# Slot-major pair features, c loaded from 32 outermost rows

## The reference

```python
x = attention(q, k, v)                      # 4608 tokens x 512
logits = x @ phi                            # 32 slots
d = softmax over tokens; slot_input = d.T @ x
slot_out = relu(slot_input[e] @ w1[e]) @ w2[e]      # 8 experts, 4 slots each
c = softmax over slots                      # 4608 x 32
y = c @ slot_out
a = y @ moe2_w1
b = y @ moe2_w2
out = ((a * b) @ moe2_w3) @ moe2_w_out
```

## Time and profile before

| | us |
|---|---|
| median of 3 runs | 410.05 |
| lowest and highest | 409.47, 415.63 |
| the profiled execution | 411.92 |
| its span, first to last instruction | 410.1 |
| PE busy in the span | 377.5 (92%) |
| POOL, DVE, ACT busy | 168.5, 170.8, 125.5 |

### The profile page before, as it was taken

The page is one execution under the profiler, slowest core; times in us unless marked ns, Lnnn a source line. Parts: engine busy times, 40 slices in busy tenths (PEclk is TensorE's granted clock), DMA queues, the critical chain, the costliest instruction groups (busy, mean ns, idle before and its releaser), DMA issues.

```text
span 410.1 us, 10206 instructions
## 1 busy us (share of the span) xinstructions
PE 377.5 (92%) x4215; PEld 272.5 (66%) x4215; DVE 170.8 (42%) x276; ACT 125.5 (31%) x246; POOL 168.5 (41%) x157
## 2 busy tenths in 40 slices
PE   1898989998999799999999999689899999989896
PEld 1887675876877586554545444467688888778775
DVE  1454465555655362530031002699723325532450
ACT  1022312321331134232233212221633435423342
POOL 1243233223322322554444420499645535754470
PEclk9999999999999999999999999899999999999999
DMA  7997999899899959586699980422214444424432
GB/s 261 371 379 245 394 397 342 284 400 390 314 359 378 378 205 339 216 340 268 247 423 419 419 336 2 86 82 95 91 44 157 177 175 176 174 102 176 177 118 102
DMA packets 38088, 102.93 MB, mean 251 GB/s; under 512 B 3552, under 2 KB 7968, under 8 KB 34208
## 3 DMA queue, kind: packets, MB, share of 16 engines
q1 hardware_dynamic: 38048, 102.34, 66.6%
HBM read 92.00 MB, written 10.32 MB: 249 GB/s over the span
## 4 chain that ended last, share of the span: by engine, by line
PE 76%; DMA 9%; issue 4%; POOL 3%; SPq 3%; DVE 3%; ACT 1%; ACTq 0%; DVEq 0%; POOLq 0%
PE psum L957 15%; PE psum L768 12%; PE psum L661 9%; PE psum L783 8%; PE psum L627 8%; DMA c_sb<-c_rows 7%; PE psum L688 5%; PE psum L925 4%; PE psum L647 4%; PE psum L674 4%; PE psum L723 3%; PE psum L699 2%; DMA pkg_sb<-in_tiles 2%; POOL feat L593 2%; SPq L509 2%
## 5 line engine op out<-in xcount | busy, mean ns | idle before, releaser
L593 POOL TENSOR_TENSOR feat<-c_sb 128x512 f32<-128x512 f32 x45 | 62.3, 1408 | 45.8 <-DMA c_sb<-c_rows 29.2
L957 PE MATMUL psum<-m_hi,feat_hi 128*128 128x512 f32 x144 | 56.5, 393 | 5.0 <-ACT out_sb L1124 3.3
L1142 DVE TENSOR_TENSOR weights_t<-psum,const_sb 128x512 f32<-128x512 f32 x72 | 46.3, 685 | 34.5 <-PE psum L627 26.8
L549 POOL TENSOR_TENSOR pkg_sb<-pkg_sb,const_sb 128x512 f32<-128x512 f32 x27 | 28.4, 1052 | 73.4 <-DMA pkg_sb<-in_tiles 73.4
L957 PE MATMUL psum<-m_hi,feat_lo 128*128 128x512 f32 x144 | 56.1, 389 | 0.0
L957 PE MATMUL psum<-m_lo,feat_hi 128*128 128x512 f32 x144 | 56.1, 389 | 0.0
L404 DVE TENSOR_TENSOR feat_lo<-feat,feat_hi 128x512 fp32r<-128x512 f32 x32 | 28.4, 889 | 60.2 <-ACT feat_hi L1092 58.2
L1092 ACT CAST feat_hi<-feat 128x512 fp32r<-128x512 f32 x45 | 27.7, 624 | 55.3 <-POOL feat L593 55.3
L567 POOL TENSOR_TENSOR w_lo<-fold_raw,w_hi 128x512 fp32r<-128x512 f32 x16 | 20.7, 1295 | 49.2 <-ACT wo_hi L1034 49.2
L627 PE MATMUL psum<-pkg_sb 64*64 64x128 f32 (+1 forms) x864 | 27.9, 267 | 10.3 <-DMA pkg_sb<-in_tiles 9.5
L976 ACT COPY state_sb<-psum 128x256 f32<-128x256 f32 x32 | 11.9, 373 | 80.1 <-PE psum L674 80.1
(11 more groups left out here) (136 smaller groups left out, 591.9 us busy)
## 6 DMA issues: line engine op xcount, KB each, us to landing
pkg_sb<-in_tiles SPq DMA_DIRECT2D x57, 256.0 KB, 7.0
pkg_sb<-in_tiles SPq DMA_DIRECT2D x24, 512.0 KB, 7.2
unit_a<-in_units SPq DMA_DIRECT2D x11, 1024.0 KB, 6.9
unit_x<-in_units SPq DMA_DIRECT2D x9, 1024.0 KB, 5.2
c_sb<-c_rows SPq DMA_DIRECT2D x36, 256.0 KB
out<-out_sb SPq DMA_DIRECT2D x36, 256.0 KB, 6.9
fold_raw<-in_fold SPq DMA_DIRECT2D x12, 512.0 KB, 7.2
unit_a<-in_units SPq DMA_DIRECT2D x12, 512.0 KB, 7.7
```

The lines of the kernel that those rows point to most:

```text
L549: nc.gpsimd.tensor_tensor(v_nat(g, t).rearrange("p (h d) -> p h d", h=HEADS), v_nat(g, t).rearrange("p (h d) -> p h d", h=HEADS), decay.un ...
L593: nc.gpsimd.tensor_tensor(feat[:, k, :], c_sb[:, s, x, :], c_sb[:, s, y, :], ALU.mult).then_inc(feat_ready, 1)
L957: last = mm(psum[:, OUT + b, :], x, y, start=(at == 0 and m == 0), stop=(at == 4 and m == 2))
L1142: tt(weights_t[:, (2 * t + odd) % 4, :].rearrange("p (k b n) -> p k b n", k=2, b=2), psum[:, odd, :].rearrange("p (k b n) -> p k b n", k=2 ...
```

## The change

The order of a feature tile's 128 rows is turned round: from four shifts of 32 slots to 32 slots of four shifts, in the tiles 0 to 3; the squares keep their order. `pair_terms` therefore reads and writes runs of four (its source steps are 0, 1 or 2 elements) where it had runs of 32. `load_c` puts the 32 slots outermost in its four loads. The tile with shift 0 now has four copies of each slot side by side, so the squares need a tile of their own in the old order: a fifth load with the shape [4 copies, 32 slots, 512 tokens]. `c_sb` grows by a tile in each buffer, the wait of POOL counts five loads, and the rows that are halved (the shift of 16 counts each pair twice) are now every fourth.

```diff
-        c_sb = place("c_sb", [P, 2, 4, CHUNK * P], at=top[1])
+        c_sb = place("c_sb", [P, 2, 5, CHUNK * P], at=top[1])
...
+        def shifted4(base, at, step, *outer):
+            return bass.AP(base.tensor, base.offset + at,
+                           [list(base.ap[0])] + [list(n) for n in outer] + [[1, SLOTS], [step, 4]])
...
-                (dst[:, 0:2 * P].rearrange("p (k i s) -> p k i s", k=2, s=SLOTS),
-                 shifted(plain, 0, (0, 2), (0, 4)), shifted(y, 1, (1, 2), (2, 4))),
-                (by_slots(dst[:, 2 * P:3 * P]), shifted(plain, 0, (0, 4)), shifted(y, 13, (1, 4))),
-                (by_slots(dst[:, 3 * P:4 * P]), shifted(x, 1, (2, 4)), shifted(y, 13, (1, 4))),
+                (dst[:, 0:2 * P].rearrange("p (k s i) -> p k s i", k=2, s=SLOTS),
+                 shifted4(plain, 0, 0, (0, 2)), shifted4(y, 1, 2, (1, 2))),
+                (dst[:, 2 * P:3 * P].rearrange("p (s i) -> p s i", s=SLOTS),
+                 shifted4(plain, 0, 0), shifted4(y, 13, 1)),
+                (dst[:, 3 * P:4 * P].rearrange("p (s i) -> p s i", s=SLOTS),
+                 shifted4(x, 1, 2), shifted4(y, 13, 1)),
                 (dst[:, 4 * P:NFEAT], shifted(plain, 0), shifted(y, 0))]
...
-        FEATURES = ((0, 1), (0, 2), (0, 3), (1, 3), (0, 0))
+        FEATURES = ((0, 1), (0, 2), (0, 3), (1, 3), (4, 4))
...
+                base = c_rows[:, bass.ds(n * (CHUNK * P), CHUNK * P)]
                 for a, (at, step) in enumerate(C_SHIFTS):
-                    base = c_rows[:, bass.ds(n * (CHUNK * P), CHUNK * P)]
                     src = bass.AP(base.tensor, base.offset + at * TOKENS,
-                                  [[step * TOKENS, 4], [TOKENS, SLOTS], [1, CHUNK * P]])
+                                  [[TOKENS, SLOTS], [step * TOKENS, 4], [1, CHUNK * P]])
                     sp.dma_start(c_sb[:, s, a, :], src).then_inc(c_loaded[s], 16)
+                src = bass.AP(base.tensor, base.offset, [[0, 4], [TOKENS, SLOTS], [1, CHUNK * P]])
+                sp.dma_start(c_sb[:, s, 4, :], src).then_inc(c_loaded[s], 16)
...
-                pool.wait_ge(c_loaded[s], (n + (2 - s)) * 32)
+                pool.wait_ge(c_loaded[s], (n + (2 - s)) * 40)
...
-    c[:, C_HALF] = np.where(np.arange(P) >= 3 * SLOTS, 0.5, 1.0)
+    c[:, C_HALF] = np.where(np.arange(P) % 4 == 3, 0.5, 1.0)
```

## The result

| | before | after |
|---|---|---|
| median, 20 runs each, us | 411.22 | 407.24 |
| lowest and highest | 408.68, 415.63 | 404.52, 409.46 |
| the profiled execution | 411.92 | 409.46 |
| its span | 410.1 | 407.6 |

The ratio of after to before is 0.9899, with a 95% interval of 0.987 to 0.9927: 4.0 us faster, 1%, which is clear of the noise and under the 2% that the prediction took as its line. The forecast was 405.8, with a range of 404.0 to 409.0 and a gain of 4.2. Of the 1.4 us between 405.8 and 407.24, 1.2 lie in the base: three runs of the kernel before gave 410.05, twenty gave 411.22.

The account below looks back on a forecast made before the run. The prediction took four DMA engines' throughput to bound the late chunks, with PE next. Loads -4.2, issue 0, DVE 0 and POOL 0 gave 410.05 - 4.2 = 405.85, rounded to 405.8 us, range 404.0 to 409.0.

Parts of the forecast that it names:

- The bound: Late chunks: throughput of four DMA engines, 328 KB each, 13.1 to 13.4 us a step; PE next with 11.83.
- The gain: Chunk stage, first to last output copy: 98.84 us down to 8 x 11.83 = 94.64, so 4.2 us.
- The wide loads: Chunk stage, four loads with 32 outermost: 402 GB/s as the output stores, 1.05 MB in 2.6 us.
- The bound of 116 GB/s: The four changed loads' bad side, from stores of c in 512 B pieces: 9.0 us a chunk.
- rival C: Loads spread but go slowly, decided near 160 GB/s; over 2% slower 2 in 100, a time between 2 in 100.
- The fifth load: Chunk stage: 262 KB on four engines at 98 GB/s, 2.7 us, hidden by PE's 11.83 us.
- In time: Chunk 3's loads: all there by about 319, POOL can use them about 322.6; about 3.5 us to spare.
- pair_terms: Build of M, runs of four: 0 on DVE (to +0.1 us a slice), 0 on POOL (to +5.5 us).
- Rival A: Build of M: POOL's runs of four are dear; gain given back 8 in 100, over 2% slower 3 in 100.
- its form with a fixed price for each run of four: POOL in pair_terms: each run a read command, 10.9 us a slice, some 55 us slower; 1 in 100.
- The gap ahead of slice 6: Build of M: PE's idle before 287.31, 1.1 us, set by DVE beside POOL's products; called the only gap left.
- rival D: More gain than the stage's, from an earlier first chunk: 405 at best; over 2% faster 2 in 100.

Follow-up runs that it names:

- loaded-up kernel: The changed kernel with its narrow fifth load issued three times, into tiles nobody reads, and waited for: 416.75 us against 411.69 for before, ratio 1.0135.
- five narrow loads: The kernel before with the fifth load alone, all five loads of a chunk with 4 outermost: 428.78 us against 411.69, ratio 1.0438.
- the lists alone: The kernel before with only the new shifted4 and pair_terms (runs of four), loads unchanged: 411.26 us against 410.55, ratio 1.0009.
- two attempts to shrink it: Changed kernel with PE's earlier first-chunk start and chunk 0's first two feature tiles made earlier: 406.25 us; also with the fifth load in four wide parts: 405.95.
- one constant: The changed kernel with PE's first-chunk wait at a count of 2 low parts instead of 5: 403.83 us against 410.55 for before, ratio 0.9842.

## Why the prediction was right

**The bound.** Held. The late steps were the throughput of four DMA engines: 13.15 us at four narrow loads, 15.84 at five, PE's 11.79 at three. The sum of bytes per engine gave 13.1 to 13.4, 15.7 to 16.0, and under 11.79.

**The gain.** 4.2 forecast. The median moved by 4.0, the stage by 4.54. The stage's term was 0.34 us too small, since the rhythm of PE was taken as the mean of two early steps, 11.86 and 11.79; the eight steps are 94.30, nearly 8 x 11.79. That the median's 4.0 lies so near to 4.2 is partly luck, as its interval reaches from 3.0 to 5.3 us.

**The wide loads.** Mis-sized. The prediction took 402 GB/s from the stores, as the row with the same piece, and so 2.6 us a chunk; measured are about 290 GB/s, 3.6 us. It cost nothing, since the sum is 8.9 us where 8.0 stood, under PE's 11.79. The bound of 116 GB/s was far off, and rival C's turning point of 160 GB/s was not reached. In the loaded-up kernel the same error was worth 0.9 us a step.

**The fifth load.** Held: hidden; without it, or in wide parts, the stage is 94.30 all the same.

**In time.** Held. The loads of chunk 3 are issued at 311.69 and their traffic ends at about 320 us, 4.7 us ahead of POOL's use at 324.73. The forecast had 3.5 us to spare; the later chunks have about 4. Issue fell from 5.60 us for the four loads of a late chunk to 2.76 and 0.58 for the five. It goes with the load on the four engines: with five narrow loads it was 8.7 to 11.0 us, with three 2.1.

**pair_terms.** Held, 0 on DVE and POOL: 741, 621 and 396 ns in the changed kernel, 743, 622 and 395 with the lists alone, against 769, 617 and 391. On DVE (`pair_u`) the three reshaped forms took 414, 412 and 276 ns on average, against 415, 420 and 277. Rival A falls with these, and so does its form with a fixed price for each run of four, by which the kernel would have been some 55 us slower.

**The gap ahead of slice 6** (rival D) stayed: PE's wait there is 0.84 us in the trace of before, where the prediction says 1.1, and 0.82 after. Of two attempts to shrink it one left it about as it was (0.88) and one made it longer (1.57). The prediction called it the only gap left in the build, and that was wrong: the chain of before also has 1.60 us of "issue" at 294.42, ahead of the first chunk, and this gap is the one that paid. The forecast didn't rest on it, as the change leaves it at 1.61.

## What to carry to other kernels

Add up the bytes that each DMA engine has to move in a loop step, and not only those of the whole step: here a load whose outermost dimension is 4 moved 98 GB/s on four engines while twelve stood idle, and the mean share of 0.4 looks like room. Compare the time of the busiest DMA engine with that of the engine that comes next; here the gain of a late step was the difference of the two, 13.15 against 11.79, and not what the faster loads would have allowed. Check a wait that counts several producers for the part that its reader needs first: here one constant brought 1.9 us of the build.

## What the runs showed of the hardware

Wide loads of c (2 KB rows, 18 KB apart, most rows read several times) moved 290 GB/s with the engines 0.87 busy, stores of the same piece 399 to 402. The narrow loads moved 98 GB/s on four engines, which is more for each engine: 24.5 against 18, or against 21 if only the busy time of the wide ones is counted.

In the chunk stage the granted clock of PE fell in the two slowed kernels only. With five narrow loads PE stands idle for 3.7 us before the last chunk, and the clock is 0.50 of full speed, the level of 1.2 GHz, in a window after it has begun again:

```profile
406.00:407.00 1.00, 0.00 (x0) 0.00 (x0) 0.98 (x1) 0.54 (x2) 1.00 (x2) 1.00 0.00 0
...
409.00:410.00 1.00, 1.00 (x4) 0.71 (x4) 0.42 (x1) 0.71 (x3) 0.81 (x1) 0.50 1.05 387
```

Its 52 products took 13.68 us, where those of the last chunk in the kernel before took 12.08. In the kernel before PE was idle for about 1.1 us a late chunk and the clock stayed at 1.00. So a late load can cost more than its lateness, here 1.6 us more for the last chunk. The same fall in two earlier chunks of that kernel cost nothing: the DMA engines set the pace there, and a step with it lasts 15.86 us (from 343.69) and one without it 15.84 (from 359.55). The loaded-up kernel has it in one chunk, the 0.50 at 375 us above.

In the build of M the clock falls in every kernel. In the kernel before PE waits 2.86 us ahead of slice 0, and the windows at 264 and 265 us stand at 0.50:

```profile
262.33 0.47 PE L925 MATMUL psum<-w_hi,pair_hi 128*128 128x512 f32 x1 [2.86 <-ACT pair_hi L1099]
...
264.00:265.00 1.00, 1.00 (x4) 0.74 (x3) 0.74 (x4) 0.00 (x0) 1.00 (x3) 0.50 0.64 117
```

A product of that slice starts 0.43 us after the one ahead of it there, and 0.23 us once the clock is back. The change leaves this as it is.
